# The batch loop of a fused attention, mixture and gated-MLP kernel, written out as straight-line code

## The chip, the cores and the metric

The kernel runs on one core of a Trainium2 chip. Its time is the device time of one execution in microseconds (us). Before the change it is 947.79 us, the median of 3 runs (945.3 to 950.71).

## The reference

Three layers follow one another for 8 batches of 576 positions, all in float32:

```python
kv = einsum('bhsd,bhse->bhde', k, v)                 # 8 heads of 64
out = einsum('bhsd,bhde->bhse', q, kv)
x = out / sqrt(mean(out*out, -1) + 1e-6) * g_norm    # then heads side by side: (8, 576, 512)

logits = x @ w_gate                                  # 4 experts, the best 2 weighted by a softmax
for e in range(4):                                   # every expert is causal attention of width 64
    scores = (x @ wq[e]) @ (x @ wk[e]).T / 8         # causal mask
    y += gate[e] * softmax(scores) @ (x @ wv[e]) @ wo[e]

h = gelu(y @ w_in);  u, v = halves of h              # 512 + 512
v_n = (v - mean) / sqrt(var + 1e-6) * g_ln
v_s = w_sg @ v_n + b_sg                              # mixes the 576 positions
result = y + (u * v_s) @ w_out
```

## The kernel before

One batch at a time passes through all five engines. Positions lie in 5 tiles of 128 (64 rows of padding ahead of the 576). Products that need more than a rounded float32 product are made of three: operands are split in a high part, written by ScalarE, and a low part, written by VectorE, and `split_product` (line 871 holds its matmul) adds high by high, high by low and low by high in PSUM.

The order of the work is written by hand in the lists `ATTENTION`, `MLP` and `MIXED`, and `PLAN` puts them together for three parts of the program:

- "pre": preparation of the weights, and the first layer (`qT`, `kv`, `o`, `x`) for batch 0;
- "loop": attention and MLP of batch i, and the first layer of batch i+1 woven between the output products of batch i. It is executed for i = 0 to 6;
- "end": attention, MLP and output of batch 7, without a next batch.

Each engine has its own instruction stream with a function `body(part, ...)` that walks through `PLAN[part]` and issues what this engine has to do for each unit. "pre" and "end" are straight code. "loop" is code of one turn inside `Fori`, a loop that the engine itself executes: it has a register with the turn, an addition, and a compare-and-branch back to the first instruction (lines 411 for the DMA queue's engine, 498 for GpSimd, 611 for ScalarE, 849 for VectorE, 1081 for TensorE). The DMA queue's engine loops 6 times, the others 7.

The engines meet through semaphores alone. There is no barrier between turns. Two PSUM tiles of two banks (`w0`, `w1`) and four of one bank (`t0` to `t3`) are handed round; TensorE raises `full[slot]` behind the last matmul of a unit, and the reader raises `free[slot]`. All semaphores only count upward, so the value waited for grows from turn to turn: in `Slots.before` it is `i * total + constant`, and in `count(b, per_batch, k)` it is `b[0] * per_batch + (b[1] * per_batch + k)`. Inside `Fori`, i is a register, so these values are computed by register instructions (the helper's lines 62, 66, 70). In "pre" and "end" they are constants, as Python has computed them. A turn begins on TensorE with the four products `("qk", (m, 0))` of 12 matmuls each, which read `wqk_s` and `xT` (named `big` in the profile); they wait until VectorE has written the low part of tile 2 of x (line 782), while the last instruction of the turn before is the transpose of tile 4 of x (line 1021).

The loads of q, k and v of batch i+2 are issued in turn i by the DMA queue's engine, as soon as TensorE has read the buffers; the output tiles are stored by the same queue.

Of the kernel before, what the change touches and what calls it, by code (L numbers as in the profile page):

```python
# [81 lines left out]
def moe_chain(nc, q, k, v, g_norm, w_gate, wq, wk, wv, wo, w_in, g_ln, w_sg, b_sg, w_out, out):  # L82
    B, H, S, HD = q.shape
# [114 lines left out]
    with ExitStack() as ctx:  # L198
# [156 lines left out]
        @block.sync  # L355
        def _(sp):
            def load_kv(b):
                for x, dst, main in ((k, kin, k_main), (v, vin, v_main)):
                    sp.dma_start(dst[PAD:P, 4 * D:NT * D].rearrange("p (h d) -> p h d", h=H),
                                 x[b, :, 0:PAD, :].rearrange("h s d -> s h d")).then_inc(kv_loaded, 16)  # L360
                    sp.dma_start(main, x[b, :, PAD:S, :].rearrange("h (p j) d -> p h (j d)", j=4)
                                 ).then_inc(kv_loaded, 16)

            def load_q(b):
                sp.dma_start(qin[PAD:P, 0, :].rearrange("p (h d) -> p h d", h=H),
                             q[b, :, 0:PAD, :].rearrange("h s d -> s h d")).then_inc(q_loaded, 16)
                for t in range(1, NT):
                    sp.dma_start(qin[:, t, :].rearrange("p (h d) -> p h d", h=H),
                                 q[b, :, P * t - PAD:P * (t + 1) - PAD, :].rearrange("h s d -> s h d")
                                 ).then_inc(q_loaded, 16)  # L370

            def store(part, i, b, ts):
                for t in ts:

                    u.wait_drained(sp, part, i, ("out", t))
                    if t == 0:
                        dst, src = out[b, 0:PAD, :], out_tile[0][PAD:P, :]
                    else:
                        dst, src = out[b, P * t - PAD:P * (t + 1) - PAD, :], out_tile[t % 2]
                    sp.dma_start(dst, src).then_inc(stored[t % 2], 16)  # L380

            sp.dma_start(wo_st, wo.rearrange("(c e) h d -> (e h) c d", e=2)).then_inc(w_loaded["wo"], 16)
            for c in range(DC):
                sp.dma_start(win_st[c], w_in[P * c:P * (c + 1), :]).then_inc(w_loaded[f"win_{c}"], 16)
            load_kv(0)
            load_q(0)
            for a in range(2):
                sp.dma_start(gnorm_c[HD * a:HD * (a + 1), :],
                             g_norm.rearrange("(p a) -> p a", a=1)).then_inc(w_loaded["gnorm"], 16)  # L390
            for c in range(DC):
                for j, w in enumerate((wq, wk)):
                    sp.dma_start(wqk_st[:, c, j, :, :],
                                 w[:, P * c:P * (c + 1), :].rearrange("e p h -> p e h")).then_inc(w_loaded["wqk"], 16)
            for c in range(DC):
                sp.dma_start(wv_st[:, c, 0:E * HD].rearrange("p (e h) -> p e h", e=E),
                             wv[:, P * c:P * (c + 1), :].rearrange("e p h -> p e h")).then_inc(w_loaded["wv"], 16)
            sp.dma_start(wv_st[:, :, E * HD:VW],
                         w_gate.rearrange("(c p) e -> p c e", p=P)).then_inc(w_loaded["wv"], 16)
            for t in range(4):  # L400
                sp.dma_start(wsg_st[t][:, PAD:SP], w_sg[P * t:P * (t + 1), :]).then_inc(w_loaded["wsg"], 16)
            sp.dma_start(wsg_st[4][0:S - 4 * P, PAD:SP], w_sg[4 * P:S, :]).then_inc(w_loaded["wsg"], 16)
            sp.dma_start(gln_c[:, :], g_ln.rearrange("(c p) -> p c", p=P),
                         allow_slow_non_contiguous=True).then_inc(w_loaded["small"], 16)
            sp.dma_start(bias_t[:, :], b_sg.partition_broadcast(P)).then_inc(w_loaded["small"], 16)
            sp.dma_start(wout_st, w_out.rearrange("(c p) n -> p c n", p=P)).then_inc(w_loaded["wout"], 16)
            u.wait_full(sp, "pre", 0, ("kv", 0))
            load_kv(1)
            u.wait_full(sp, "pre", 0, ("qT", NT - 1))
            load_q(1)  # L410
            with sp.Fori(0, B - 2) as i:

                u.wait_full(sp, "loop", i, ("kv", 0))
                load_kv(i + 2)
                store("loop", i, i, (0, 1))
                u.wait_full(sp, "loop", i, ("qT", NT - 1))
                load_q(i + 2)
                store("loop", i, i, (2, 3, 4))
            store("loop", B - 2, B - 2, range(NT))
            store("end", 0, B - 1, range(NT))  # L420
            for r in range(2):
                sp.wait_ge(stored[r], 16 + B * n_stored[r])

        @block.gpsimd
        def _(pool):
# [69 lines left out]
                                                ALU.mult).then_inc(gated_ready, 1)  # L495

            body("pre", None, (0, 0))
            with pool.Fori(0, B - 1) as i:
                body("loop", (i, 0), (i, 1))
            body("end", (0, B - 1), None)  # L500

# [1 line left out]
        def _(act):  # L503
# [104 lines left out]
                        vhat_high(VHAT_AFTER[U])  # L608

            body("pre", 0, None, (0, 0))  # L610
            with act.Fori(0, B - 1) as i:
                body("loop", i, (i, 0), (i, 1))
            body("end", 0, (0, B - 1), None)

# [1 line left out]
        def _(dve):  # L616
# [229 lines left out]
            dve.wait_ge(w_loaded["small"], 2 * 16)  # L846
            dve.wait_ge(consts_ready, 1)
            dve.wait_ge(w_lo, 4)
            with dve.Fori(0, B - 1) as i:
                body("loop", i, (i, 0), (i, 1))  # L850
            body("end", 0, (0, B - 1), None)

# [1 line left out]
        def _(pe):  # L854
# [223 lines left out]
            body("pre", 0, None, (0, 0))  # L1078

            pe.wait_ge(w_lo, 3)  # L1080
            with pe.Fori(0, B - 1) as i:
                body("loop", i, (i, 0), (i, 1))
            body("end", 0, (0, B - 1), None)

# [23 lines left out]
```

## Time and profile before

| | |
|---|---|
| time, median of 3 runs | 947.79 us (945.3 to 950.71) |
| span of the profiled execution, first to last instruction | 941.3 us; its own time is not recorded beside it |
| TensorE matmuls | 893.4 us busy, 95% |
| TensorE weight loads (beside the matmuls) | 768.0 us, 82% |
| VectorE | 459.9 us, 49% |
| ScalarE | 413.0 us, 44% |
| GpSimd | 178.7 us, 19% |
| bytes read and written in HBM | 35.19 MB and 9.44 MB, 47 GB/s |

The profile is one execution, taken by the hardware. "PE" is TensorE's matmuls and "PEld" its weight loads, DVE is VectorE, ACT ScalarE, POOL GpSimd, SP the DMA queue's engine. A q behind an engine's name (PEldq) marks instructions that its sequencer executes itself: register arithmetic, semaphore instructions, branches. They aren't counted as busy. "issue" as the cause of a wait means that nothing which the profile shows released the engine. The granted clock of TensorE is a share of 2.4 GHz: 1.00 is that, 0.50 is 1.2 GHz.

### The profile page before, as it was taken

To read this page: it belongs to the slowest core of one execution; us is meant where nothing else is said; L and a number is where in the kernel's file an instruction comes from. 1 tells how busy PE (TensorE), PEld (TensorE's weight loads), DVE (VectorE), ACT (ScalarE), POOL (GpSimd) and SP (SyncE) were. 2 spreads that over 40 slices of the span, in tenths; PEclk is the share of its full clock that TensorE was granted. 3 is DMA by queue.
4 is the path that set the end of the run, shared out by engine and by line. 5 is a ranking of instruction groups with operands and counts; after the bars stand their busy time and mean duration, and the time that the engine had idled before them with its cause. 6 is when DMAs were issued, how large, how long until landed. Compare 5 with 4: busy or idle time off the path is not lost.

```text
span 941.3 us, 19467 instructions
## 1 busy us (share of the span) xinstructions
PE 893.4 (95%) x7009; PEld 768.0 (82%) x7009; DVE 459.9 (49%) x1218; ACT 413.0 (44%) x972; POOL 178.7 (19%) x209
## 2 busy tenths in 40 slices
PE   7599998999989999899998999989998999999997
PEld 3597887979878798878988789887897879897796
DVE  1657633475335743277332772337633475337730
ACT  0656523373335633365243652336423463346521
POOL 0400233002420033102330022300242002410130
PEclk9999999999999999999999999999999999999999
DMA  9930303003030033000230021300304000000001
GB/s 261 258 77 2 102 7 97 1 1 102 18 85 1 1 101 71 32 1 17 86 90 13 1 67 36 91 13 1 102 6 97 1 1 1 17 35 1 1 1 51
DMA packets 77645, 45.83 MB, mean 49 GB/s; under 512 B 54592, under 2 KB 70976, under 8 KB 77568
## 3 DMA queue, kind: packets, MB, share of 16 engines
q1 hardware_dynamic: 77568, 44.63, 18.2%
q8 instruction: 69, 1.13, 0.5%
q14 instruction: 8, 0.07, 0.0%
HBM read 35.19 MB, written 9.44 MB: 47 GB/s over the span
## 4 chain that ended last, share of the span: by engine, by line
PE 83%; DVE 6%; issue 5%; ACT 4%; POOL 0%; DMA 0%; POOLq 0%; ACTq 0%; DVEq 0%
PE w L871 37%; PE t L871 20%; PE t L925 6%; PE t L1013 4%; PE w L910 3%; PE t L941 3%; PE w L1058 2%; ACT probs L566 2%; PE t L1002 2%; PE t L957 2%; PE w L978 2%; PE t L1021 2%; DVE probs L707 2%; DVE neg_max L686 1%; ACT yT L583 1%
## 5 line engine op out<-in xcount | busy, mean ns | idle before, releaser
L871 PE MATMUL t<-big,wqk_s 128*128 128x288 f32 x768 | 112.6, 303 | 17.1 <-issue 17.1
L871 PEld LDWEIGHTS t<-big,wqk_s 128*128 128x128 f32 x768 | 105.6, 193 | 18.9 <-issue 18.5
L871 PE MATMUL w<-wout_s,big 128*128 128x512 f32 x480 | 119.2, 397 | 1.6 <-DVE big L735 1.6
L871 PE MATMUL w<-wsgT_s,big 128*128 128x288 f32 x768 | 110.8, 300 | 0.0
L871 PEld LDWEIGHTS w<-wsgT_s,big 128*128 128x128 f32 x768 | 103.2, 189 | 5.2 <-issue 5.2
L871 PEld LDWEIGHTS w<-wout_s,big 128*128 128x128 f32 x480 | 89.3, 189 | 22.0 <-DVE big L735 2.1
L566 ACT ACTIVATE probs<-w,neg_max 128x64 f32<-128x64 f32 (+4 forms) x160 | 83.0, 527 | 46.3 <-DVE neg_max L686 45.5
L487 POOL TENSOR_TENSOR var_eps<-bn,eps_t 128x1 f32<-128x1 f32 x40 | 14.8, 369 | 464.1 <-DVE bn L723 463.0
L579 ACT ACTIVATE work<-t 128x384 f32<-128x384 f32 (+3 forms) x160 | 63.1, 448 | 47.9 <-PE t L925 47.3
L925 PE MATMUL t<-ident,probs 128*128 128x128 f32 x480 | 72.4, 282 | 8.5 <-DVE probs L707 7.7
L837 DVE SCALAR_TENSOR_TENSOR work<-w,gln_c,bias_t 128x576 f32<-128x576 f32 x32 | 26.2, 818 | 111.2 <-PE w L871 111.2
L600 ACT ACTIVATE big<-work 128x576 fp32r<-128x576 f32 x32 | 22.0, 687 | 132.5 <-POOL work L494 132.5
L494 POOL TENSOR_TENSOR work<-work,qT_uT 128x576 f32<-128x576 f32 x32 | 56.2, 1755 | 123.8 <-DVE work L837 123.8
L686 DVE TENSOR_REDUCE neg_max<-w 128x1 f32<-128x64 f32 (+4 forms) x160 | 73.9, 484 | 5.4 <-PE w L910 4.4
L606 ACT ACTIVATE work<-w 128x512 f32<-128x512 f32 x40 | 23.9, 597 | 118.3 <-PE w L871 118.3
L925 PEld LDWEIGHTS t<-ident,probs 128*128 128x128 f32 x480 | 52.0, 140 | 27.9 <-issue 18.6
L941 PE MATMUL t<-work,vals 128*64 128x128 f32 x960 | 70.1, 281 | 0.8 <-DVE work L820 0.8
L775 DVE TENSOR_REDUCE ss<-squares 128x8 f32<-128x512 f32 x40 | 27.4, 685 | 85.8 <-ACT squares L538 85.8
L468 POOL TENSOR_TENSOR rms_inv<-ms,neg_half 128x8 f32<-128x8 f32 x40 | 65.7, 1642 | 3.1
L707 DVE TENSOR_SCALAR probs<-probs,row_inv,gate 128x64 f32<-128x64 f32 (+4 forms) x160 | 64.2, 444 | 2.9
L910 PE MATMUL w<-big 64*128 64x288 f32 (+4 forms) x576 | 64.1, 328 | 0.0
L871 PE MATMUL w<-wo_s,yT 128*128 128x512 f32 x240 | 62.7, 402 | 0.0
(105 smaller groups left out, 1406.3 us busy)
## 6 DMA issues: line engine op xcount, KB each, us to landing
kin<-in_k_dram SPq DMA_DIRECT2D x8, 1024.0 KB, 6.1
vin<-in_v_dram SPq DMA_DIRECT2D x8, 1024.0 KB, 8.7
qin<-in_q_dram SPq DMA_DIRECT2D x32, 256.0 KB, 4.5
out_dram<-work SPq DMA_DIRECT2D x32, 256.0 KB, 2.1
staged_win<-in_moe_w_in_dram SPq DMA_DIRECT2D x4, 512.0 KB, 6.5
probs<-in_moe_w_sg_dram SPq DMA_DIRECT2D x4, 288.0 KB, 3.8
kin<-in_k_dram SPq DMA_DIRECT2D x8, 128.0 KB, 2.8
vin<-in_v_dram SPq DMA_DIRECT2D x8, 128.0 KB, 6.8
```

Source lines behind the costliest of these rows:

```text
L468: nc.gpsimd.tensor_tensor(rms_inv[:, j, :], ms[:, j, :], neg_half[:, 0:H], ALU.pow).then_inc(rms_ready, 1)
L494: nc.gpsimd.tensor_tensor(gt_tile[j % 2], gt_tile[j % 2], qT_uT[:, j, PAD:SP], ALU.mult).then_inc(gated_ready, 1)
L566: exps = nc.scalar.activation(probs[:, j % 2, a, PAD:PAD + K], ps[slot][:, o:o + K], ACT.Exp, bias=neg_max[:, j, a:a + 1], accum_out=row_s ...
L579: give(nc.scalar.activation(pT[:, j % 2, a, P * lo:P * hi], x[:, 0:P * (hi - lo)], ACT.Copy), V)
L686: nc.vector.tensor_reduce(neg_max[:, n, a:a + 1], ps[slot][:, o:o + K], AX_X, ALU.max, negate=True).then_inc(max_ready, 1)
L707: last = nc.vector.tensor_scalar(x, x, row_inv[:, n, a:a + 1], gate[:, t, 2 * e + a:2 * e + a + 1], ALU.mult, ALU.mult)
L775: nc.vector.tensor_reduce(ss[:, j, :], sq_tile.rearrange("p (h d) -> p h d", h=H), AX_X, ALU.add).then_inc(ss_ready, 1)
L871: last = nc.tensor.matmul(o, stationary(hs, c), mv(hm, c), start=c == of[0] and p == 0, stop=c == of[-1] and p == len(PASSES) - 1)
L910: last = nc.tensor.matmul(ps[slot][:, o:o + w], big2[rows, hs, e, P * t:P * (t + 1)], big2[rows, hm, EP + e, PAD + k0:PAD + k0 + w], start ...
L925: last = nc.tensor.transpose(x[:, P * (b - lo):P * (b - lo + 1)], probs[:, n % 2, a, P * b:P * (b + 1)], ident[:, :])
L941: last = nc.tensor.matmul(x[HD * a:HD * (a + 1), P * e:P * (e + 1)], vals[:, b, w:w + HD], pT[:, n % 2, a, P * b:P * (b + 1)], start=b == ...
L1013: last = nc.tensor.matmul(x[:, P * c:P * (c + 1)], qT_uT[:, c, P * j:P * (j + 1)], kvd[:, c, :], start=True, stop=True)
```

## The change

The five `Fori` loops become Python loops, so that the body's code stands in each engine's stream seven times (six on the DMA queue's engine), one copy behind the other, between "pre" and "end". i is then a number: every wait value and every address is a constant, and the counters and branches are gone. The order of the instructions on each engine, the buffers and the semaphores waited for are the same.

```diff
@@ -408,7 +408,7 @@
-            with sp.Fori(0, B - 2) as i:
+            for i in range(B - 2):
                 u.wait_full(sp, "loop", i, ("kv", 0))
                 load_kv(i + 2)
@@ -495,7 +495,7 @@
-            with pool.Fori(0, B - 1) as i:
+            for i in range(B - 1):
                 body("loop", (i, 0), (i, 1))
@@ -608,7 +608,7 @@
-            with act.Fori(0, B - 1) as i:
+            for i in range(B - 1):
                 body("loop", i, (i, 0), (i, 1))
@@ -846,7 +846,7 @@
-            with dve.Fori(0, B - 1) as i:
+            for i in range(B - 1):
                 body("loop", i, (i, 0), (i, 1))
@@ -1078,7 +1078,7 @@
-            with pe.Fori(0, B - 1) as i:
+            for i in range(B - 1):
                 body("loop", i, (i, 0), (i, 1))
```

## Rows read from the trace of the kernel before

**Rows 1.** The page: span, and busy time, share and instructions of engines.
```profile
span 941.3 us, 19467 instructions
...
PE 893.4 (95%) x7009; PEld 768.0 (82%) x7009; DVE 459.9 (49%) x1218; ACT 413.0 (44%) x972; POOL 178.7 (19%) x209
```

**Rows 2.** The page: the chain that ended last, shares by engine.
```profile
PE 83%; DVE 6%; issue 5%; ACT 4%; POOL 0%; DMA 0%; POOLq 0%; ACTq 0%; DVEq 0%
```

**Rows 3.** TensorE's waits: line, releaser: us in total, times, longest us.
```profile
PE t L871 <- issue: 17.1, 6, 3.0
PE t L925 <- DVE probs L707: 7.7, 23, 0.5
```

**Rows 4.** Timeline of TensorE, each turn's start: start us, us, what [idle before].
```profile
50.14 6.59 PE L871 MATMUL t<-big,wqk_s 128*128 128x288 f32 x48
...
162.42 8.03 PE L871 MATMUL t<-big,wqk_s 128*128 128x288 f32 x48 [2.84 <-issue]
...
276.22 6.58 PE L871 MATMUL t<-big,wqk_s 128*128 128x288 f32 x48 [2.90 <-issue]
...
388.15 6.58 PE L871 MATMUL t<-big,wqk_s 128*128 128x288 f32 x48 [2.50 <-issue]
...
500.49 7.97 PE L871 MATMUL t<-big,wqk_s 128*128 128x288 f32 x48 [2.88 <-issue]
...
614.38 6.58 PE L871 MATMUL t<-big,wqk_s 128*128 128x288 f32 x48 [3.02 <-issue]
...
726.87 6.58 PE L871 MATMUL t<-big,wqk_s 128*128 128x288 f32 x48 [3.01 <-issue]
...
836.07 6.56 PE L871 MATMUL t<-big,wqk_s 128*128 128x288 f32 x48
```

**Rows 5.** Loop lines' branches: ns min/median/max, first and last start us.
```profile
L1081 PEldq COMPARE_BRANCH  x7: 83/3732/3873, 158.5 to 835.2; - x7
...
L611 ACTq COMPARE_BRANCH  x7: 40/45/45, 159.7 to 836.4; - x7
...
L849 DVEq COMPARE_BRANCH  x7: 50/56/67, 160.6 to 837.3; - x7
```

**Rows 6.** Timeline, TensorE's last group ahead of two seams.
```profile
158.99 0.60 PE L1021 MATMUL t<-ident,work 128*128 128x128 f32 x4
...
835.72 0.60 PE L1021 MATMUL t<-ident,work 128*128 128x128 f32 x4
```

**Rows 7.** Windows behind two gaps; PEclk, the granted clock, follows the busy times.
```profile
core 0: us, PE busy (x) PEld busy (x) DVE busy (x) ACT busy (x) POOL busy (x), PEclk, DMA share, GB/s
...
162.42:166.00 3.58, 3.58 (x16) 3.58 (x17) 0.00 (x0) 0.30 (x1) 0.00 (x0) 0.55 0.02 5
...
276.22:280.00 3.78, 3.78 (x28) 3.78 (x29) 0.46 (x1) 0.73 (x2) 0.00 (x0) 1.00 0.02 4
```

**Rows 8.** Wait helper, line 62, on TensorE's sequencer: ns min/median/max, starts.
```profile
L62 PEldq ALU_OP  x308: 32/32/32, 56.3 to 827.5; - x154
L62 PEldq EVENT_SEMAPHORE  x265: 51/51/663, 29.1 to 912.8; - x133
```

**Rows 9.** Timeline of TensorE, the same transposes in turn 7 and batch 8.
```profile
775.73 0.88 PE L925 MATMUL t<-ident,probs 128*128 128x128 f32 x6
...
884.93 0.87 PE L925 MATMUL t<-ident,probs 128*128 128x128 f32 x6
```

**Rows 10.** Timeline of ScalarE, batch 8's table load ahead of its first Exp.
```profile
843.10 1.28 ACT L566 ACT_TABLE_LOAD   x1
```

**Rows 11.** Waits of the DMA queue's engine: us in total, times, longest us.
```profile
SPq L380 <- ACT work L606: 479.3, 40, 90.7
```

**Rows 12.** The page's DMA queues of instructions: packets, MB, share.
```profile
q8 instruction: 69, 1.13, 0.5%
q14 instruction: 8, 0.07, 0.0%
```

## The prediction, on record before the changed kernel was run

> **What bounds the kernel now.** I read the page first: its busy table, then the chain that ended last, then who waited for whom, then the starts of the turns in the order of time. In the busy table TensorE is at work 95% of a span of 941.3 us, while VectorE has 49% and ScalarE 44% [rows 1]. The chain agrees: 83% of the time that sets the end is TensorE's, 6% VectorE's, 4% ScalarE's, and 5% is "issue", time in which the engine waited for nothing that the profile shows [rows 2]. A kernel like this gets faster only where TensorE's own time shrinks or its gaps close, so the next view is the list of its waits. Two entries in it come back turn after turn: 7.7 us in 23 short waits for VectorE's scaled probabilities, and 17.1 us in just 6 waits put down to "issue", at most 3.0 us each, all ahead of a line-871 matmul that reads wqk_s [rows 3].
>
> Six waits, and the loop over the batches has seven turns, so six times its branch jumps back. The timeline shows where they are. Each turn begins with 48 matmuls of that kind. They begin at 50.14, 162.42, 276.22, 388.15, 500.49, 614.38, 726.87 us and, for the eighth batch, which is written out behind the loop, at 836.07 [rows 4]. The first has no gap before it (the loop is entered), the next six have gaps of 2.84, 2.90, 2.50, 2.88, 3.02 and 3.01 us (together 17.15), and the last has none (the loop is left) [rows 4]. The gap stands where the branch is taken and nowhere else.
>
> The records of the loops' own lines say the same. TensorE's compare-and-branch appears 7 times with a minimum of 83 ns and a median of 3732 ns; ScalarE's and VectorE's stay at 45 and 56 ns, taken or not [rows 5]. So it is TensorE's instruction stream that stands still for 3.7 us at a jump back. Of these about 2.9 us reach the matmuls (17.15/6), as the sequencer is about a microsecond ahead of the array: the array is busy with the last transposes until 158.99 + 0.60 = 159.59 us and starts again at 162.42 [rows 4, 6].
>
> The gap has a second price. In two of the six turns the first 48 matmuls take 8.03 and 7.97 us, in the other turns 6.58 [rows 4]. In the first 3.58 us after the gap at 162.42 the granted clock is 0.55, that is mostly the lower level, 1.2 GHz; after the gap at 276.22 it is 1.00, 2.4 GHz [rows 7]. TensorE had stood idle ahead of both. Gaps of 2.90, 3.01 and 3.02 us left the clock up and gaps of 2.84 and 2.88 did not, so which gap costs it cannot be read from its length [rows 4].
>
> **The change part by part.** It takes away the five loops' branches and counters, turns each wait value computed from the counter into a constant, and repeats the body's code seven times (six on the DMA queue's engine).
>
> 1. The taken branch of TensorE. The clean measure is from start to start. The turn that leaves the loop takes 836.07 − 726.87 = 109.20 us. The six turns before it take 726.87 − 50.14 = 676.73 us, and six of the clean kind would take 655.20: the difference is 21.5 us [rows 4]. By parts: 17.15 of gaps; (8.03 − 6.58) + (7.97 − 6.58) = 2.8 of low clock; and 6 × 0.25 = 1.5, as a gap is counted from the modelled end of the last transpose, while without a gap the next matmul starts 0.25 us before that end (835.72 + 0.60 against 836.07) [rows 4, 6]. Together 21.5. All of it is on the path, as TensorE is what is waited for. What is late next? The seam at 836.07 answers that: it is this very seam, same body before it, same start of attention behind it, constants in the waits, no jump, and nothing is late there. So I take the whole 21.5.
>
> The rule that explains it is in the Trainium skill, "Runtime: NRT & Kernel Launch", section "Instruction fetch mechanics": instructions are fetched ahead only in sequence, and a taken branch whose target is not in the window held forces a fetch before execution goes on. The trace agrees, with 3.7 us against 0.083. A rule that would speak against it is in "Advanced Engine Details and Errata" of the same Trainium skill, section "ISA Cache": TensorE holds 128 KB of instructions. With 7009/8 = 876 matmuls and as many weight loads a turn, of 64 bytes by that skill, the body is about 112 KB and ought to be held, and its branch cheap; the 3.7 us would then be a wait of another kind, which could outlive the loop (the second rival below).
>
> 2. Register arithmetic in the waits. In the loop one helper line alone executes 308 ALU instructions of 32 ns on TensorE's sequencer, 44 a turn; constants come as waits of 51 ns (265 of the same line) [rows 8]. Both are ahead of the array. What they cost on the path is read by laying the written-out batch over turn 7: the first transposes of the last pair of heads' probabilities (line 925, six) start at 775.73, that is 48.86 us after the turn's start, and in the written-out batch at 884.93, also 48.86 us after it [rows 4, 9]. That stretch holds the softmax chains of VectorE and ScalarE as well, and up to it the two do the same work. Lower end of the cost: 0. Bound on a gain: all of the 7.7 us that TensorE waits for VectorE [rows 3]. Bound on a loss: 7 × 44 instructions that become 19 ns longer, 5.9 us, if nothing hid them. The row nearest to it says 0.00, so I take nothing for it; the cover is the matmuls already queued.
>
> 3. Table load of ScalarE. In the written-out batch the table for Exp is loaded just ahead of the first Exp, 1.28 us at 843.10, and not at the top of the body [rows 10]. Seven turns may get that place. TensorE is then in 48 matmuls of the value projection that don't read the result, and step 2's comparison includes it: 0. Without that cover it would be 6 × 1.28 = 7.7 us.
>
> 4. Branches of the other engines, and the DMA queue. 45 and 56 ns each in engines that are half idle [rows 1, 5]; the DMA queue's engine waits 479 us for ScalarE's output tiles alone [rows 11]: 0. Each of its transfers is issued at the same place in its order; turns that are 3.5 us shorter do not starve one that waits for buffers, not for the memory.
>
> 5. More code to fetch. TensorE passes through its body's code once per turn already: queue q8 brought 69 packets, 1.13 MB, and no more than 6 waits came of it, all at the branch [rows 3, 12]. Straight code asks for no more than that. The other engines hold their loops: q14 brought 8 packets in all [rows 12]. The loop's and the last batch's code are about two of eight batches, so written out they need about 8 × 8/2 = 32 (estimate), 24 more. In turn 1, where their code comes for the first time, the turn takes 162.42 − 50.14 = 112.28 us, and the fourth, where none of their code is new, 500.49 − 388.15 = 112.34 [rows 4]. So 24 × 0.
>
> Sum: −21.5 us against a profiled span of 941.3 gives a span of 919.8. The profiled execution's total time is not recorded beside its span; the timed median, 947.8, lies 6.5 us above the span, and I keep these 6.5: 926.3 us.
>
> **The rivals.** A: the branch's time goes, but other executions have other numbers of slow starts. If the median run had none, the gain is 17.15 + 1.5 = 18.7 and the time 929.1; if all six, it is 18.7 + 6 × 1.4 = 27.1, and 920.7. For it: the three timed runs spread over 5.4 us, as much as four such starts. This widens the forecast more than it opposes it.
> B: what the branch shows is really a dependence (the last x tile, VectorE at line 782, or a drained buffer) that stays when the branch is gone. Time 947.8. Against it: the seam at 836.07 has the same dependences and no gap [rows 4, 6].
> C: the register work is in the chain of VectorE and ScalarE after all, and the waits for the probabilities go as well: another 7.7, 918.6. Against it: the 48.86 of both [rows 4, 9].
> D, slower: the code of the smaller engines, now streamed, arrives late. Price at a branch's 3.7 us for each of the 24 extra packets: 89 us, less 21.5, so 1015 us. It decides above 21.5/24 = 0.9 us exposed per packet. For it: ScalarE and VectorE are close behind TensorE in attention, 23 waits of it. Against it: turn 1, and the same engines' straight code in the last batch, show nothing.
>
> **How the numbers follow.** The forecast with A's spread has 0.84; C 0.05; B 0.04; D 0.04; 0.03 for a partial gain, with stalls at new page borders taking back more than half. About 0.5%, 4.7 us, is what a measurement of this kernel can tell from no change. Faster by more than that: 0.84 + 0.05 + 0.02 = 0.91; within it: 0.05; slower: 0.04. The range is A's, 920.7 to 929.1, widened to C's end below and by 3 us above (half of step 2's bound on a loss): 918.5 to 932.
>
> **What would show it.** TensorE's waits have no "issue" entry of 17 us; the starts of the eight batches lie 109.2 us apart; no stretch behind a seam has a clock of 0.55; the waits for the probabilities remain near 7.7 us; q14 has some 30 packets instead of 8, q8 somewhat fewer than 69. The prediction is wrong if a gap of over 1 us stays at the seams (B), if turns are 108 us or less (C), or if ScalarE or VectorE shows new issue gaps and the turns are longer than 112 us (D).

## The result, and the profile after

The written-out kernel takes 923.3 us (median of 4 runs, 922.6 to 923.4), against 949.2 us for the kernel before on the same chip (median of 4, 945.3 to 950.7). The ratio is 0.9746, with a 95% interval from 0.9713 to 0.9778. The forecast was 926.3 us with a range from 918.5 to 932.

The page of the kernel after, its span, busy table and queues of instructions, answers to [rows 1, 12]:

```profile
span 921.6 us, 17530 instructions
...
PE 889.8 (97%) x7009; PEld 765.3 (83%) x7009; DVE 460.2 (50%) x1218; ACT 410.9 (45%) x971; POOL 176.3 (19%) x209
...
q8 instruction: 57, 0.93, 0.4%
q14 instruction: 23, 0.19, 0.1%
```

The number of matmuls is the same and the span is 19.7 us shorter. About 1900 executed instructions are gone, the counters and most of the register arithmetic. TensorE's queue of instructions (q8) brought 57 packets, fewer than the 69 of the loop; the other engines' (q14) brought 23 instead of 8.

TensorE's waits after the change (line, releaser: us in total, times, longest us), against [rows 3]:

```profile
PE t L925 <- DVE probs L707: 6.8, 16, 0.6
PE w L966 <- DMA work<-in_moe_wo_dram: 4.6, 1, 4.6
```

The entry of 17.1 us with the cause "issue" is gone. The starts of the eight batches, from the same timeline as [rows 4]:

```profile
50.41 6.59 PE L871 MATMUL t<-big,wqk_s 128*128 128x288 f32 x48
...
159.84 6.56 PE L871 MATMUL t<-big,wqk_s 128*128 128x288 f32 x48
...
269.23 6.56 PE L871 MATMUL t<-big,wqk_s 128*128 128x288 f32 x48
...
378.64 6.56 PE L871 MATMUL t<-big,wqk_s 128*128 128x288 f32 x48
...
488.10 6.56 PE L871 MATMUL t<-big,wqk_s 128*128 128x288 f32 x48
...
597.52 6.56 PE L871 MATMUL t<-big,wqk_s 128*128 128x288 f32 x48
...
706.98 6.56 PE L871 MATMUL t<-big,wqk_s 128*128 128x288 f32 x48
...
816.41 6.56 PE L871 MATMUL t<-big,wqk_s 128*128 128x288 f32 x48
```

No start has a gap before it, and none of the groups of 48 takes 8 us. A turn is (816.41 − 50.41)/7 = 109.43 us long on average, where the one clean turn before took 109.20 and the six others 111.9 to 113.9 [rows 4]. The windows behind two of the seams, in the form of [rows 7]:

```profile
core 0: us, PE busy (x) PEld busy (x) DVE busy (x) ACT busy (x) POOL busy (x), PEclk, DMA share, GB/s
159.84:163.40 3.56, 3.56 (x30) 3.56 (x29) 1.21 (x2) 1.56 (x4) 0.00 (x0) 1.00 0.20 74
...
488.10:491.70 3.60, 3.60 (x30) 3.60 (x29) 1.21 (x2) 1.60 (x4) 0.00 (x0) 1.00 0.20 73
```

The granted clock is 1.00, the upper level, where it was 0.55 behind the gap at 162.42. From 50.41 to 816.41 are 766.00 us, from 50.14 to 836.07 were 785.93: so 19.9 us were won between the first start and the last, and 0.3 lost ahead of the first, which together are the span's 19.7. The written-out last batch takes 921.6 − 816.4 = 105.2 us, exactly as before.

### The profile page after: what moved, and what is told of

It reads as the page before. It is cut to its first block, busy times and chain, and to the rows that moved or that the text cites. A ratio compares the mean times of both kernels' runs of the same rounds, so it can differ in the third digit from the quotient of the medians.

```text
span 921.6 us, 17530 instructions
## 1 busy us (share of the span) xinstructions
PE 889.8 (97%) x7009; PEld 765.3 (83%) x7009; DVE 460.2 (50%) x1218; ACT 410.9 (45%) x971; POOL 176.3 (19%) x209
## 4 chain that ended last, share of the span: by engine, by line
PE 81%; DVE 10%; ACT 7%; issue 1%; POOL 0%; DMA 0%; POOLq 0%; ACTq 0%; DVEq 0%
PE w L871 38%; PE t L871 19%; ACT probs L566 5%; PE t L925 4%; PE t L1013 4%; PE w L910 3%; DVE neg_max L686 3%; PE w L1058 3%; DVE probs L707 2%; PE t L941 2%; PE t L1002 2%; PE t L957 2%; PE w L978 2%; PE t L1021 2%; ACT work L579 1%; DVE yT L812 1%
## 5 line engine op out<-in xcount | busy, mean ns | idle before, releaser
L871 PE MATMUL t<-big,wqk_s 128*128 128x288 f32 x768 | 109.6, 298 | 0.0
L871 PEld LDWEIGHTS t<-big,wqk_s 128*128 128x128 f32 x768 | 102.8, 188 | 0.4
L941 PEld LDWEIGHTS t<-work,vals 128*64 128x64 f32 x960 | 51.0, 136 | 15.8 <-issue 13.7
```

What stands on the lines that cost most here:

```text
L871: last = nc.tensor.matmul(o, stationary(hs, c), mv(hm, c), start=c == of[0] and p == 0, stop=c == of[-1] and p == len(PASSES) - 1)
L941: last = nc.tensor.matmul(x[HD * a:HD * (a + 1), P * e:P * (e + 1)], vals[:, b, w:w + HD], pT[:, n % 2, a, P * b:P * (b + 1)], start=b == ...
```

## The experiments

Medians and ratios are against the kernel before, run on the same chip between them. The first four ran on one chip (before: 947.94 us, 13 runs), the next three on another (before: 949.77, 7 runs). Five more kernels, further down, ran once each and are read by their traces.

| kernel | us, median (range) | ratio (95% interval) |
|---|---|---|
| TensorE alone written out | 923.19 (921.95 to 925.08) | 0.9736 (0.9691 to 0.9781) |
| the other four written out | 946.91 (942.42 to 950.32) | 0.9984 (0.9957 to 1.0011) |
| all loops, hint on TensorE's branch | 924.21 (921.26 to 926.65) | 0.9738 (0.9688 to 0.9788) |
| TensorE's loop with two turns a pass | 933.85 (931.77 to 934.49) | 0.9846 (0.9802 to 0.9891) |
| all written out, again | 924.76 (923.28 to 926.09) | 0.9748 (0.9706 to 0.9790) |
| all written out, fewer waits | 923.79 (922.42 to 926.88) | 0.9744 (0.9700 to 0.9789) |
| TensorE alone, fewer waits | 923.27 (921.51 to 925.03) | 0.9724 (0.9680 to 0.9768) |

**TensorE's loop alone, and all but TensorE's.**

```diff
-            with pe.Fori(0, B - 1) as i:
+            for i in range(B - 1):
```

> TensorE's loop alone is written out; ScalarE, VectorE, GpSimd and the DMA queue keep their loops. Theory (the whole gain is TensorE's taken branch with the gap and the slow starts behind it): the time of the fully written-out kernel, 923 us within 2, starts of the batches 109.4 us apart, no issue gap at the seams. Rival 1 (constants and missing branches on the other engines carry a share): some 5 to 10 us above that. Rival 2 (a dependence at the seam, set free only when all streams are straight): near 949.

The opposite half has the same edit in the streams of ScalarE, VectorE, GpSimd and the DMA queue (there with B - 2), and not in TensorE's.

> The opposite half: the four other loops are written out, TensorE keeps its own. Theory: the time of the kernel before, 949 us within 2, six issue gaps of about 2.9 us, and starts of turns 112 to 114 us apart. Rival 1 (the other engines carry a share): 940 to 945 us. Rival 3 (their streamed code costs something, which TensorE's gain hides): 951 or more.

One line on TensorE gives all of the gain, 923.2 us. The four others together give nothing that these times can tell from zero, 946.9. In the second kernel TensorE's list of waits still begins with the gaps, and its branch still stands still (waits as in [rows 3], and the loop line's record as in [rows 5]):

```profile
PE t L871 <- issue: 15.5, 6, 2.8
```

```profile
L1081 PEldq COMPARE_BRANCH  x7: 83/3558/3732, 158.9 to 839.2; - x7
```

Two starts of batches in the first kernel are 489.39 − 380.13 = 109.26 us apart:

```profile
380.13 6.56 PE L871 MATMUL t<-big,wqk_s 128*128 128x288 f32 x48
...
489.39 6.56 PE L871 MATMUL t<-big,wqk_s 128*128 128x288 f32 x48
```

That is some 0.15 us less than with all five loops written out (109.4), so the straight code of the smaller engines costs a little; more on this below. The first turn of this execution began at the lower clock, although no loop's branch stands ahead of it; its first 48 matmuls took 8.28 us instead of 6.59:

```profile
50.63 8.28 PE L871 MATMUL t<-big,wqk_s 128*128 128x288 f32 x48
```

**The loop kept, the branch told ahead.** The hint is one instruction at the top of each turn.

```diff
-            with pe.Fori(0, B - 1) as i:
+            with nc.Fori(0, B - 1, engines=[mybir.EngineType.PE], hint_back_edge=True) as i:
```

TensorE's loop line, and the page's queue of its instructions:

```profile
L1081 PEldq BRANCH_PREFETCH_HINT  x7: 31/31/45, 51.5 to 709.8; - x7
...
L1081 PEldq COMPARE_BRANCH  x7: 80/216/252, 163.5 to 818.8; - x7
```

```profile
q8 instruction: 15, 0.25, 0.1%
```

The branch takes 216 ns instead of 3732, the gaps are gone, and the time is that of straight code. The dependences at the seam are the same with the hint and without it. So the 3.7 us were a fetch: no dependence and no draining of TensorE was in them. From the second start to the eighth (164.33 and 819.63 us) a turn takes 655.30/6 = 109.22 us, which is the 109.20 of the one clean turn before.

The packets say more. With the hint 15 of them (0.25 MB) come in the whole execution, so the loop's code stays from turn to turn. The written-out kernel has six more copies of the body and 57 − 15 = 42 more packets, seven a copy. Without the hint it is 69 − 15 = 54 more, nine for each of the six jumps back: the whole body was read again in each turn.

**Two turns a pass.**

```diff
-            with pe.Fori(0, B - 1) as i:
-                body("loop", i, (i, 0), (i, 1))
+            with pe.Fori(0, (B - 1) // 2) as h:
+                for r in range(2):
+                    i = h * 2 + r
+                    body("loop", i, (i, 0), (i, 1))
+            body("loop", B - 2, (0, B - 2), (0, B - 1))
```

> TensorE's loop has two turns per pass, three passes, and the seventh turn is written out behind it: two taken branches instead of six. Theory: gaps of about 2.9 us at two seams only (behind turns 2 and 4), the time 923.3 + 2/6 of the 25.9 us of difference = 932 us, within 2.5. If instead the size of a body set the price of a branch (twice the code, twice the fetch), each of the two gaps would be about 6 us and the time 938.

```profile
274.51 8.12 PE L871 MATMUL t<-big,wqk_s 128*128 128x288 f32 x48 [2.71 <-issue]
...
385.23 6.56 PE L871 MATMUL t<-big,wqk_s 128*128 128x288 f32 x48
...
497.13 8.13 PE L871 MATMUL t<-big,wqk_s 128*128 128x288 f32 x48 [2.48 <-issue]
```

Two gaps of 2.7 and 2.5 us at the two seams that still have a taken branch, none at the seam inside a pass, and 933.9 us against 932 expected. Twice the body did not double a gap, which fits a fetch whose first code, and not its whole length, is waited for. Both gaps were followed by a slow start (8.12 and 8.13 us).

**How long a body may be.** Four runs, one execution each, read only the branch. The first leaves out the third term of the split products, the second also the second term; both compute less than the kernel before. A body counts 1867 instructions in the kernel before, matmuls, weight loads and the sequencer's own together.

```diff
-PASSES = ((HI, HI), (HI, LO), (LO, HI))
+PASSES = ((HI, HI), (HI, LO))          # the second kernel: ((HI, HI),)
```

> The kernel before with its five loops, but the split products leave out the last of their three terms (low part of the stationary operand), so TensorE's body has 1539 instructions instead of 1867. Read is the record of TensorE's taken branch, not the time. Theory (a fetch, needed because the body with what is fetched ahead does not stay in the store that TensorE fetches from): the price depends on the body's size and falls to about 0.1 us at some size below the present one; this may or may not be small enough. Rival (every taken branch of TensorE costs 3.7 us): 3.5 to 3.8 us.

> As the run beside it, but only the first of the three terms is left: a body of 1211 instructions. Theory: the taken branch costs 0.1 us. Rival: 3.5 to 3.8 us here too.

The third and the fourth fill the body with two terms up again, on TensorE, in the loop's part:

```diff
+                    if part == "loop" and kind == "u":
+                        for _ in range(80):        # the other kernel: 130
+                            pe.wait_ge(consts_ready, 1)
```

> The run with two of the three terms (body of 1539 instructions, taken branch 0.21 us), filled up with 160 semaphore instructions on TensorE that never have to wait, to a body of 1699. Read is the record of the taken branch and the number of q8 packets. Theory: size decides, and the step is somewhere between 1539 and 1867; a store of eight blocks of 256 instructions, of which the body with its ragged ends takes one more than its size, would still hold this one: 0.2 us and some 12 packets. Rival (it was not the size but the work left out that made the branch cheap): 0.2 us in this run and in the next.

> As the run beside it with 260 such instructions, a body of 1799, above seven blocks of 256. Theory: with its ragged ends and the block fetched ahead it no longer stays: branch 3 us or more, some 60 q8 packets. Rival (not the size): 0.2 us.

The record of the taken branch and the q8 line of the page, first with 1539 instructions in the body, then 1211, 1699, and 1799:

```profile
q8 instruction: 12, 0.20, 0.1%
...
L1081 PEldq COMPARE_BRANCH  x7: 76/208/239, 143.5 to 695.5; - x7
```

```profile
q8 instruction: 9, 0.15, 0.1%
...
L1081 PEldq COMPARE_BRANCH  x7: 76/207/239, 141.2 to 653.4; - x7
```

```profile
q8 instruction: 13, 0.21, 0.1%
...
L1084 PEldq COMPARE_BRANCH  x7: 76/208/239, 160.3 to 795.2; - x7
```

```profile
q8 instruction: 40, 0.66, 0.3%
...
L1084 PEldq COMPARE_BRANCH  x7: 83/244/4147, 171.1 to 888.1; - x7
```

Up to 1699 instructions the loop is read once and the branch costs 0.2 us. At 1799 the jumps alternate: one by one the six taken branches cost 0.24, 3.78, 0.23, 4.00, 0.24 and 4.15 us. The packets agree: 40 are 27 more than at 1699, nine for each of the three dear jumps, as many as each jump brought at 1867. "3 us or more" was right for half of its branches, so 1799 lies on the border and not behind it. At 1867 all six cost 3.3 us and more. Since the same work left out is cheap at 1699 and not at 1799, it is the size that decides. The times of the four are not comparable with the others, as they compute less, and the filling holds the matmuls up.

**The same on another engine.**

```diff
                 store("loop", i, i, (2, 3, 4))
+                for _ in range(1400):
+                    sp.wait_ge(consts_ready, 1)
```

> The kernel before, with 1400 waits on a semaphore that has long been raised behind the DMA queue's last store of each turn, two to an instruction; its loop body grows from some 60 to some 760 instructions, its order stays. Theory (a long body costs a fetch at the branch on any engine): the record of this engine's taken branch rises from 45 ns to 3 us or more, and the time stays near 948, as this engine waits for ScalarE anyway. Rival (the price belongs to TensorE, whose queue of matmuls has to run empty): 45 to 60 ns.

The DMA queue's loop line around its first jump back, in this kernel and then in the kernel before:

```profile
L411 SPq COMPARE_BRANCH  x1: 59/59/59, 207.6 to 207.6; - x1
L411 SPq FUSED_REGOPS  x1: 55/55/55, 210.2 to 210.2; - x1
```

```profile
L411 SPq COMPARE_BRANCH  x1: 54/54/54, 160.5 to 160.5; - x1
L411 SPq FUSED_REGOPS  x1: 50/50/50, 160.8 to 160.8; - x1
```

By its wording the expectation failed: the branch's record stays at 48 to 59 ns. The price is there all the same, behind the branch: the next instruction starts 210.2 − 207.6 = 2.6 us later, before it was 0.3, and so at all five jumps (2.5 to 2.7). A long body costs on this engine too, and the record of the branch alone would have hidden it. This body has 746 instructions, less than half of what stayed on TensorE; where the border lies on this engine was not looked for. The time, 950.7 us in one run beside 950.8 for the kernel before, shows it to be off the path there. The page of this kernel has 53 packets on q14 instead of 8.

**The 0.2 us that a turn became longer.**

> The fully written-out kernel once more, as the measure for the two runs beside it on the same chip: 923.3 us within 1, starts of the batches 109.4 us apart.

Its turns are 109.4 us apart, as expected. Two executions took 923.3 and 923.8 us with a mean clock of 1.000 and 0.998, two 925.8 and 926.1 with 0.996, so the median of 924.76 is 1.5 above the expected one.

Both kernels with fewer waits have this edit, in the written-out kernel and in the one where TensorE's loop alone is written out:

```diff
-                    for g in range(len(T_GROUPS[t])):
-                        for a in range(2):
-                            u.wait_drained(pe, part, i, ("t", n, a, g))
                     u.wait_drained(pe, part, i, ("v", t))
+                    for a in range(2):
+                        u.wait_drained(pe, part, i, ("t", n, a, len(T_GROUPS[t]) - 1))
```

> The fully written-out kernel, in which TensorE's weighted_values waits for the value tile first and then only for the last group of transposed probabilities of each head; the earlier group is in the same slot, so its count is lower and the wait for it is implied. Theory on the 0.2 us that each turn lost behind the transposes of the last scores (two semaphore instructions in a row, begun only once VectorE's last copy has ended): the distance from that copy's end to the product's start falls from 0.26 to about 0.05 us, turns from 109.41 to 109.2, the time by 1.4 us to about 922. Rival (the 0.2 us are the late copy itself, so VectorE's): no change, 923.3.

> The same two changed waits, with only TensorE's loop written out and the other four kept. In the run with TensorE alone written out the turns were 109.26 us apart, 0.15 less than with all five. Theory (both differences are in the waits that constants bring: one on TensorE, one in the packed waits of ScalarE and VectorE, which the kept loops avoid): turns of about 109.05 us, the time 920.5 within 1 apart from slow starts of the first turn. Rival: 109.26 again and 922.

VectorE's last two copies of transposed probabilities and the product that reads them, in turn 7 of the kernel before, of the kernel after, and of the one with fewer waits:

```profile
778.25 0.76 DVE L820 COPY work<-t 128x256 f32<-128x256 f32 x2 [1.82 <-PE t L925]
...
779.06 1.31 PE L941 MATMUL t<-work,vals 128*64 128x128 f32 x20
```

```profile
758.37 0.76 DVE L820 COPY work<-t 128x256 f32<-128x256 f32 x2 [1.83 <-PE t L925]
...
759.38 1.31 PE L941 MATMUL t<-work,vals 128*64 128x128 f32 x20
```

```profile
757.56 0.76 DVE L820 COPY work<-t 128x256 f32<-128x256 f32 x2 [1.82 <-PE t L925]
...
758.46 1.31 PE L940 MATMUL t<-work,vals 128*64 128x128 f32 x20
```

From the copies' end to the product's start are 779.06 − 779.01 = 0.05 us in the loop, 759.38 − 759.13 = 0.25 with constants, 758.46 − 758.32 = 0.14 with fewer of them. Between the two stand the sequencer's waits, here around that copy, first in the kernel before and then in the one after:

```profile
L70 PEldq EVENT_SEMAPHORE  x2: 51/51/51, 778.4 to 778.8; - x2
```

```profile
L70 PEldq EVENT_SEMAPHORE  x2: 51/51/51, 759.2 to 759.3; - x2
```

In the loop they have begun before the copy ends at 779.01; with constants both begin behind its end at 759.13, one after the other. Half of the expected 0.2 us came back with one of them taken away, with turns of 109.3 us:

```profile
268.90 6.56 PE L871 MATMUL t<-big,wqk_s 128*128 128x288 f32 x48
...
378.18 6.56 PE L871 MATMUL t<-big,wqk_s 128*128 128x288 f32 x48
```

With TensorE alone written out the same edit takes 109.26 to 489.87 − 380.71 = 109.16 us:

```profile
380.71 6.56 PE L871 MATMUL t<-big,wqk_s 128*128 128x288 f32 x48
...
489.87 6.56 PE L871 MATMUL t<-big,wqk_s 128*128 128x288 f32 x48
```

The theory was right in the place and too large by two: one semaphore instruction was saved, and one that now holds two waits still stands between the copy and the product. The second expectation missed: 109.16 us a turn and 923.3 us (921.5 and 922.1 in the two executions without a slow first turn), where 109.05 and 920.5 within 1 were expected; the time is nearer to the rival's 922. The ranges behind the medians, 924.76, 923.79 and 923.27, overlap; these differences are read from the traces and not from the times. No version is shown faster than the written-out kernel by the medians. The ones that keep TensorE's loop with a hint, or the loops of the four other engines, reach the same time.

TensorE's constants do not cost 0.2 us on balance. With TensorE alone written out (the turn begins at 707.94), the copy and the product in turn 7 are:

```profile
759.17 0.76 DVE L820 COPY work<-t 128x256 f32<-128x256 f32 x2 [1.82 <-PE t L925]
...
760.18 1.31 PE L941 MATMUL t<-work,vals 128*64 128x128 f32 x20
```

The product follows the copy's end by the same 0.25 us, but the copy starts 51.23 us into the turn, where it is 51.38 in the kernel before and 51.39 in the one after. So TensorE's constants win 0.15 us ahead of the copy (one of its short waits for the probabilities, 0.20 us at 33.9 us into the turn, is gone) and lose 0.20 behind it. With all five written out the 0.15 is lost again. The place can be seen: VectorE's maxima and ScalarE's first Exp behind them, in the kernel after and with TensorE alone written out:

```profile
748.64 1.42 DVE L686 TENSOR_REDUCE neg_max<-w 128x1 f32<-128x576 f32 x2
...
749.51 0.74 ACT L566 ACTIVATE probs<-w,neg_max 128x576 f32<-128x576 f32 x1 [2.62 <-DVE neg_max L686]
```

```profile
749.53 1.41 DVE L686 TENSOR_REDUCE neg_max<-w 128x1 f32<-128x576 f32 x2
...
750.31 0.74 ACT L566 ACTIVATE probs<-w,neg_max 128x576 f32<-128x576 f32 x1 [2.53 <-DVE neg_max L686]
```

From the one to the other are 0.87 us against 0.78, and about as much (0.88 against 0.79) is lost at the same place 5.4 us earlier. The kernel before and the one with the hint have 0.78 too, so the distance goes with the loops of the four engines. No run here changed ScalarE's waits, so that they are the cause is not shown.

## Why the prediction was right

**Where the time was.** Right. The taken branch of TensorE, six times, and no other engine: shown by writing out each half alone. That it is a fetch of code, which the prediction took from the row of 3732 against 83 ns and from the rule, is shown by the hint.

**Step 1, the seams.** Right in the mechanism and in size for the profiled execution: 21.5 us forecast. Between the starts 19.9 were measured, and the 1.6 that are missing arose inside the turns (step 2). The kernel with the hint shows the seams by themselves: it keeps the loop, and its turns of 109.22 us are the clean turn's 109.20. The clean turn that leaves the loop was the right measure, because it is the changed kernel's seam, already in the old trace.

**Step 1's clock term, and the way from span to median.** This is what was mis-sized. I kept 6.5 us between the profiled span and the timed median as if they lay around the kernel. In the runs on record now, each with its span, between 1.7 and 2.1 us lie around it. The rest, some 4.6 us, was inside: the profiled execution had two slow starts, a typical one more time at the lower clock. The 13 runs of the kernel before on one chip go from a span of 940.1 us with a mean clock of 0.996 to 949.3 with 0.985. The clock's difference of 0.011 is 0.011 × 2 × 945 = 21 us more at the lower level, which costs half, 10 us; measured are 9.2. If all 4.6 us go with the change, it gives 21.5 − 1.6 + 4.6 = 24.5 us, where the medians differ by 25.9 (the median before moved by 1.4 itself, from 947.8 to 949.2, with a fourth run).

No trace of a median execution of the kernel before was kept, but the kernel with the long body on the DMA queue's engine has the same work on TensorE and was profiled with a span of 948.7 us, 7.4 longer. It has slow starts behind four of its six gaps, two of them these (the others 8.13 and 8.12 us):

```profile
279.10 8.13 PE L873 MATMUL t<-big,wqk_s 128*128 128x288 f32 x48 [2.93 <-issue]
...
617.90 9.32 PE L873 MATMUL t<-big,wqk_s 128*128 128x288 f32 x48 [3.00 <-issue]
```

Over the usual 6.58 they cost 7.4 us, 4.6 more than the two of the kernel before, so not every one is worth 1.4, as rival A had them. Some 2.9 us more lie at its beginning: the clock was 0.50 from 48 to 52 us, the first turn began at 52.37 instead of 50.14 and its first 48 matmuls took 7.30 instead of 6.59. That part has nothing to do with the branch. It appears in executions with straight code on TensorE as well (8.28 us above), and how the typical 4.6 us divide between the two is not known. This was rival A, and it should have been the centre: a profile at the fast end of the timed runs says that its clock is not the typical one.

That the forecast came as close as 3.0 us owes something to luck: a gain put 4.6 us too low by this term and 1.6 too high by step 2 partly cancel. And the result's 923.3 is itself at the fast end: all four of its executions had a clock of 1.00, while the same kernel run again took 923.3 to 926.1.

**Step 2, constants in place of registers.** Forecast 0, measured +0.23 us a turn, 1.6 in all, inside the bound of 5.9 given for it (which counted the 44 register instructions a turn of line 62 and not the 14 of line 70). The comparison's 48.86 us held in the changed kernel too, but it was not a proof that nothing happens: by then TensorE's constants have won 0.15 us and the other engines' straight code has lost as much. The loss that is left begins at 52 us into the turn, and I had stopped ahead of it. What the runs put in its place: waits against constants are packed two in one semaphore instruction, and on TensorE two such instructions begin only when the copy has ended, where the loop's have begun before. The prediction priced an instruction by its length (19 ns more) and not by its place behind the event. TensorE's spot costs 0.20 us and its constants win 0.15 before it, so it loses 0.06 a turn on balance (109.26 against 109.20). The rest, some 0.15 us, is with the four other engines, as it is absent where their loops are kept; it shows at ScalarE's Exp behind VectorE's maxima, and its cause stays open.

**Steps 3 and 4, the table load and the small engines.** Forecast 0, and the time with the four others alone written out shows none that can be told from it (0.9984, 0.9957 to 1.0011). The traces do show the 0.15 us a turn, 1 us in all.

**Step 5 and rival D, code streamed by small engines.** Right in the main: 23 packets (forecast 30 or so), and no stall of the 0.9 us a packet that D needed; writing out the four engines alone left the time where it was. That a part of the open 0.15 us a turn is late code is not excluded. On TensorE, "straight code asks for no more" was right for the present body: 57 packets instead of 69. It would be wrong for a body that stays.

**Rival B** fell with the two runs of halves and with the hint. The rule of the Trainium skill on which it leaned, "Advanced Engine Details and Errata", section "ISA Cache" (128 KB on TensorE), does not decide this case by itself: of a body of 1867 instructions nothing stays without the hint and all of it with one, and bodies up to 1699 stay without. **Rival C** fell, though a little of it came true: the waits for the probabilities went from 7.7 to 6.8 us and from 23 to 16, one fewer a turn, and not to 0.

## What to carry to other kernels

Look for "issue" waits that come as often as a loop jumps back, and compare the turn that leaves the loop with the others: the difference is what the loop costs. If the engine that bounds the kernel has a long body, write out this engine's loop alone, give its branch a prefetch hint, or shorten the body until it stays; all three reached a branch of 0.2 us or none (the third only in kernels that compute less), and the other engines' loops may remain. A comparison of two stretches that comes out at 0.00 can hold a gain and a loss of the same size; change one engine at a time to see them. Before carrying a gain from a profile to a median, compare the profiled run's span and clock with those of the timed runs.

## What the runs showed of the hardware

- TensorE's taken branch costs 0.21 us with bodies of 1211, 1539 and 1699 instructions, by turns 0.24 and 3.8 to 4.1 with 1799, and 3.3 to 3.9 with 1867. A body of twice that pays the same (3.3 and 3.6 us). Every dear jump of the bodies of 1799 and 1867 brought nine packets.
- With a prefetch hint the body of 1867 instructions is not even read again: 15 packets for the whole execution instead of 69.
- On the DMA queue's engine a body of 746 instructions pays too: 2.6 us, behind the branch's record and not in it.
- A wait that begins only behind the event costs about 0.1 us: 0.05, 0.14 and 0.25 us from copy to product with none, one and two such instructions.
- Gaps in TensorE's work from 2.4 to 3.0 us were followed by the lower clock in some turns (2, 4 and 4 of six in three executions) and not in others; the shortest that was is 2.37 us, the longest that was not 3.02. The spread of the kernel before, 942 to 952 us over all runs, goes with its clock, 0.996 to 0.985.
